# Centroid similarities of a clustered attention: centroids as stationary operand in four column groups instead of queries and keys

## What is computed

```
q_assign = argmax(q_n . c_n)      # per token, over 16 centroids; k_assign the same for keys
mask     = q_assign[i] == k_assign[j]
scores   = where(mask, scale * q k^T, -1e9)
attn     = softmax(scores);   out = attn v
```

## Time and profile before

| what | value |
|---|---|
| median of three runs | 680.38 us (678.81 to 681.3) |
| the profiled execution, its own time | 680.13 us |
| its span, first to last instruction | 678.3 us |
| mean granted TensorE clock | 0.995 of full speed |
| TensorE matmuls busy (PE) | 661.5 us, 98% |
| TensorE weight loads busy (PEld) | 635.9 us, 94% |
| VectorE busy (DVE) | 382.3 us, 56% |
| ScalarE busy (ACT) | 321.7 us, 47% |
| GpSimd busy (POOL) | 191.7 us, 28% |

### The profile page before, as it was taken

One profiled execution on the slowest core, in us unless ns is written; L12 is line 12 of the kernel. 1 busy time (PEld: TensorE's weight loads), 2 busy tenths in 40 slices (PEclk: granted clock), 3 DMA queues, 4 the chain that ended last, 5 costly groups with the idle time before them and its releaser, 6 DMA issues.

```text
span 678.3 us, 11306 instructions
## 1 busy us (share of the span) xinstructions
PE 661.5 (98%) x4050; PEld 635.9 (94%) x4050; DVE 382.3 (56%) x650; ACT 321.7 (47%) x619; POOL 191.7 (28%) x140
## 2 busy tenths in 40 slices
PE   7899899999999998999999999999999999999998
PEld 6889799999999997889999999999999999999997
DVE  6889798989899895443212212312378336661142
ACT  4787778787787884344202102202478125520010
POOL 5568254554525854106200000200243000060000
PEclk8999999999999999999999999999999999999999
DMA  6584745537473611102100000100421000000022
GB/s 217 104 196 127 182 101 119 144 76 173 79 185 79 145 47 47 47 0 94 63 1 0 1 1 0 46 0 1 140 86 55 16 1 1 1 1 1 0 94 94
DMA packets 16976, 46.92 MB, mean 69 GB/s; under 512 B 3024, under 2 KB 5072, under 8 KB 16944
## 3 DMA queue, kind: packets, MB, share of 16 engines
q1 hardware_dynamic: 16944, 46.48, 25.9%
HBM read 24.15 MB, written 3.15 MB: 40 GB/s over the span
## 4 chain that ended last, share of the span: by engine, by line
PE 95%; DVE 2%; ACT 1%; DMA 1%; issue 1%; SPq 0%
PE ps L459 20%; PE ps L457 20%; PE ps L458 20%; PE ps L497 9%; PE ps L505 5%; PE ps L489 5%; PE ps L506 5%; PE ps L490 5%; PE ps L471 3%; PE ps L512 2%; DMA kb<-oh_rows 1%; PE ps L707 1%; PE ps L480 1%; PE ps L640 1%; ACT x_t L780 0%
## 5 line engine op out<-in xcount | busy, mean ns | idle before, releaser
L780 ACT ACTIVATE pt_hi<-ps 128x384 fp32r<-128x384 f32 x192 | 85.0, 489 | 42.9 <-PE ps L497 42.0
L1100 DVE TENSOR_TENSOR pt_lo<-ps,pt_hi 128x384 fp32r<-128x384 f32 x192 | 97.3, 548 | 9.6 <-ACT pt_hi L780 8.3
L1073 DVE TENSOR_REDUCE neg_max<-ps 128x1 f32<-128x768 f32 x96 | 91.1, 950 | 20.0 <-PE ps L490 19.4
L811 ACT ACTIVATE prob<-ps,neg_max 128x768 f32<-128x768 f32 x96 | 86.8, 904 | 6.3 <-DVE neg_max L1073 6.3
L894 ACT ACTIVATE g_s<-ps 128x384 fp32r<-128x384 f32 x48 | 23.6, 492 | 138.9 <-PE ps L459 138.9
L459 PE MATMUL ps<-u_s,ch_s 128*128 128x384 f32 (+1 forms) x256 | 85.5, 334 | 0.0
L457 PE MATMUL ps<-u_s,ch_s 128*128 128x384 f32 (+1 forms) x256 | 85.5, 334 | 0.0
L458 PE MATMUL ps<-u_s,ch_s 128*128 128x384 f32 (+1 forms) x256 | 85.5, 334 | 0.0
L497 PE MATMUL ps<-ident,prob 128*128 128x128 f32 x576 | 82.4, 277 | 0.5 <-DVE pt_lo L1100 0.4
L497 PEld LDWEIGHTS ps<-ident,prob 128*128 128x128 f32 x576 | 66.5, 142 | 10.0 <-issue 2.3
L489 PE MATMUL ps<-ka,qa 128*128 128x384 f32 x192 | 70.9, 369 | 5.1 <-DMA kb<-oh_rows 3.0
(11 more groups left out here) (147 smaller groups left out, 1374.0 us busy)
## 6 DMA issues: line engine op xcount, KB each, us to landing
stage<-ch_dram SPq DMA_DIRECT2D x9, 768.0 KB, 4.4
qa<-pair_s SPq DMA_DIRECT2D x30, 192.0 KB, 3.0
ka<-pair_s SPq DMA_DIRECT2D x30, 192.0 KB, 4.0
raw<-q_dram SPq DMA_DIRECT2D x8, 384.0 KB, 4.4
raw<-k_dram SPq DMA_DIRECT2D x8, 384.0 KB, 4.6
raw_v<-v_dram SPq DMA_DIRECT2D x8, 384.0 KB, 4.3
out_dram<-act_u SPq DMA_DIRECT2D x16, 192.0 KB, 1.9
qb<-pair_s SPq DMA_DIRECT2D x15, 192.0 KB, 3.4
```

What stands on the lines that cost most here:

```text
L780: return act.activation(o, i, ACT.Copy)
L811: act.activation(prob[:, slot, :].rearrange("p (c k) -> p c k", c=2), ps[:, 2 * slot:2 * slot + 2, 0:HS], ACT.Exp, bias=neg_max[:, s:s + 1 ...
L1073: dve.tensor_reduce(neg_max[:, s:s + 1], ps[:, 2 * slot2:2 * slot2 + 2, 0:HS], AX.XY, ALU.max, negate=True).then_inc(s_max, 1)
L1100: dve.tensor_tensor(pt_lo[at], ps[:, 4 + u, 0:HS].rearrange("p (k q) -> p k q", k=HT), pt_hi[at], ALU.subtract).then_inc(s_pt_lo, 1)
```

## The change

The similarities of a pair are computed with the centroids as the stationary operand (32 columns) and the queries or keys as moving operand (384 columns). Four such matmuls make up a pair: two sides, two halves of the tokens. Each writes its own 32 partitions of bank 7, and so uses its own group of 32 columns of the array. The result is centroid by token; ScalarE copies it to `sim_rows`, and three transposes bring it back to token by centroid in bank 7. The matmuls go to step 0 and the transposes to step 1, both behind what TensorE does there. [...] Argmax number 0 moves to step 1, numbers 1 and 2 stay in step 3. The one-hot rows are ordered by side first and then by head, so the setup has four small memsets where it had eight. Pair 0's own similarities at the start keep their form, with other addresses.

```diff
+                cen_p = sb(a1, "cen_p", [P, 2 * C], F32)
+                sim_rows = sb(a1, "sim_rows", [P, HS], F32)
...
             def oh_in(p, j):
...
-                    r = j * D + side * 2 * C
+                    r = side * D + j * 2 * C
...
+            def centroids_of(p, first=False):
+                if not first:
+                    pool.wait_ge(s_cen_t, 4)
+                    pool.wait_ge(s_sim_pe, p - 1)
+                pool.tensor_tensor(cen_p[:], cen_t[:].rearrange("p b c -> p (b c)")[:, bass.ds(p * 2 * C, 2 * C)],
+                                   one[:].broadcast_to([P, 2 * C]), ALU.mult).then_inc(s_cen_p, 1)
...
                 if scaled:
                     scale_q(p + 2)
+                    centroids_of(p + 2)
...
             scale_q(1)
+            pool.wait_ge(s_cen_t, 2)
+            centroids_of(1, first=True)
             split_v(0, 0, first=True)
...
-            def sims(p, side, src=raw, bank=7, first=False):
-
-                if side == 0 and not first:
-                    pe.wait_ge(s_oh_rows, p)
-                    pe.wait_ge(s_cen_t, 4)
-                    pe.wait_ge(s_qk_c, p)
-                groups = ps[:, bank, 0:24 * C].rearrange("p (t j s c) -> p t j s c", t=NT, j=2, s=2)
-                centroids = cen_t[:].rearrange("p b c -> p (b c)")[:, bass.ds(p * 2 * C, 2 * C)]
-                for t in range(NT):
-                    mm = pe.matmul(groups[:, t, :, side, :], src[:, side, t * P:(t + 1) * P],
-                                   centroids.rearrange("p (j c) -> p j c", j=2), start=True, stop=True)
-                if side == 1 or first:
-                    mm.then_inc(s_sims, 1)
+            def sims(p):
+
+                pe.wait_ge(s_oh_rows, p)
+                pe.wait_ge(s_cen_p, p)
+                pe.wait_ge(s_qk_c, p)
+                for side in range(2):
+                    for half in range(2):
+                        r = (2 * half + side) * 2 * C
+                        mm = pe.matmul(ps[r:r + 2 * C, 7, 0:HS], cen_p[:], raw[:, side, half * HS:(half + 1) * HS],
+                                       start=True, stop=True)
+                mm.then_inc(s_sim_pe, 1)
+
+            def sims_transpose(p):
+
+                pe.wait_ge(s_sim_rows, p)
+                for t in range(HT):
+                    mm = pe.transpose(ps[:, 7, t * P:(t + 1) * P], sim_rows[:, t * P:(t + 1) * P], ident[:])
+                mm.then_inc(s_sims, 1)
...
-                    if s == 3 and not last:
-                        sims(p + 1, 0)
+                    if s == 0 and not last:
+                        sims(p + 1)
...
-                    if s == 3 and not last:
-                        sims(p + 1, 1)
+                    if s == 1 and not last:
+                        sims_transpose(p + 1)
...
+                    if s == 0 and not last:
+                        act.wait_ge(s_sim_pe, p + 1)
+                        copy(sim_rows[:], ps[:, 7, 0:HS]).then_inc(s_sim_rows, 1)
                     if s == 7 and not last:
...
                     if not last:
-                        for step in {3: (0, 1, 2), 4: (3,), 6: (4,)}.get(s, ()):
+                        for step in {1: (0,), 3: (1, 2), 4: (3,), 6: (4,)}.get(s, ()):
                             argmax(p + 1, step)
```

More of the change, by code:

```diff
@@ L80, in clustered_mixer @@
                 pt_lo = sb(a1, "pt_lo", [P, 2, NT, HS], F32R)
-                onehot = sb(a1, "onehot", [P, NT, 2, 2, 2 * C], BF16)
+                onehot = sb(a1, "onehot", [P, HT, 2, 2, 2, 2 * C], BF16)
                 oh_rows = sb(a1, "oh_rows", [P, S], F32R)
@@ L137, in clustered_mixer @@
         s_cen_t = sem("s_cen_t")
+        s_cen_p = sem("s_cen_p")
+        s_sim_pe = sem("s_sim_pe")
+        s_sim_rows = sem("s_sim_rows")
         s_sims = sem("s_sims")
@@ L459, in product, with sims_first @@
                 return pe.matmul(o, a_hi, b_hi, start=False, stop=stop)
-            def sims(p, side, src=raw, bank=7, first=False):
-                if side == 0 and not first:
-                    pe.wait_ge(s_oh_rows, p)
-                    pe.wait_ge(s_cen_t, 4)
-                    pe.wait_ge(s_qk_c, p)
-                groups = ps[:, bank, 0:24 * C].rearrange("p (t j s c) -> p t j s c", t=NT, j=2, s=2)
-                centroids = cen_t[:].rearrange("p b c -> p (b c)")[:, bass.ds(p * 2 * C, 2 * C)]
-                for t in range(NT):
-                    mm = pe.matmul(groups[:, t, :, side, :], src[:, side, t * P:(t + 1) * P],
-                                   centroids.rearrange("p (j c) -> p j c", j=2), start=True, stop=True)
-                if side == 1 or first:
-                    mm.then_inc(s_sims, 1)
+            def sims_first(side, bank):
+                groups = ps[:, bank, 0:24 * C].rearrange("p (t h s j c) -> p t h s j c", t=HT, s=2, h=2, j=2)
+                for t in range(NT):
+                    mm = pe.matmul(groups[:, t % HT, t // HT, side, :, :], raw0[:, side, t * P:(t + 1) * P],
+                                   cen_t[:, 0, 0:2 * C].rearrange("p (j c) -> p j c", j=2), start=True, stop=True)
+                mm.then_inc(s_sims, 1)
[13 more added lines that the diff above has]
+                    mm = pe.transpose(ps[:, 7, t * P:(t + 1) * P], sim_rows[:, t * P:(t + 1) * P], ident[:])
+                mm.then_inc(s_sims, 1)
             def oh_transpose(bank=7):
@@ L480, in oh_transpose @@
                     mm = pe.transpose(rows[:, t * P:(t + 1) * P],
-                                      onehot[:, t, :, :, :].rearrange("p j s c -> p (j s c)"), identb[:])
+                                      onehot[:, t % HT, t // HT, :, :, :].rearrange("p s j c -> p (s j c)"), identb[:])
                 mm.then_inc(s_oh_t, 1)
@@ L594, in _ @@
             pe.wait_ge(s_q0_scaled, 1)
-            sims(0, 0, src=raw0, first=True)
+            sims_first(0, bank=7)
             pe.wait_ge(s_raw_k0, 16)
-            sims(0, 1, src=raw0, bank=4, first=True)
+            sims_first(1, bank=4)
             for side in range(2):
@@ L799, in mask_rows_first @@
                 act.wait_ge(s_oh_t, 2)
-                act.activation(kb[D:D + C, 0, :], ps[2 * C:3 * C, 5, 0:HS].bitcast(BF16), ACT.Copy,
+                act.activation(kb[D:D + C, 0, :], ps[D:D + C, 5, 0:HS].bitcast(BF16), ACT.Copy,
                                scale=BIG, bias=-BIG).then_inc(s_koh, 1)
@@ L842, in pair @@
                         rows_out(p + 1)
-            act.wait_ge(s_oh_zero, 9)
+            act.wait_ge(s_oh_zero, 5)
             query_rows_first()
@@ L985, in _ @@
             dve.memset(onehot[:], 0.0).then_inc(s_oh_zero, 1)
[L986 to L989, removed]
+            for side in range(2):
+                rows = slice(side * D, (side + 1) * D)
+                dve.memset(oh_scale[rows, :], BIG if side else 1.0).then_inc(s_oh_zero, 1)
+                dve.memset(oh_bias[rows, :], -BIG if side else 0.0).then_inc(s_oh_zero, 1)
             for c in range(C):
@@ L1025, in _ @@
             normalised(1, 1)
-            hot = onehot[:].rearrange("p t j s c -> p (t j) s c")
+            hot = onehot[:].rearrange("p t h s j c -> p (t h) s j c")
             def argmax_first(side):
-                r = slice(12 * side, 12 * side + 12)
-                sim = ps[:, 4 if side else 7, 0:24 * C].rearrange("p (n s c) -> p n s c", s=2, c=C)[:, :, side, :]
-                shape = [P, 12, C]
+                at1, at2 = (m[:].rearrange("p (s t n) -> p s t n", s=2, t=NT)[:, side] for m in (am1, am2))
+                sim = ps[:, 4 if side else 7, 0:24 * C].rearrange("p (t s n c) -> p t s n c", t=NT, s=2, c=C)[:, :, side]
+                shape = [P, NT, 2, C]
                 dve.wait_ge(s_sims, side + 1)
-                dve.tensor_reduce(am1[:, r], sim, AX.X, ALU.max).then_inc(s_am0, 1)
+                dve.tensor_reduce(at1, sim, AX.X, ALU.max).then_inc(s_am0, 1)
                 dve.wait_ge(s_am0, 4 * side + 1)
-                dve.tensor_tensor(sim, sim, am1[:, r].unsqueeze(2).broadcast_to(shape),
+                dve.tensor_tensor(sim, sim, at1.unsqueeze(3).broadcast_to(shape),
                                   ALU.is_ge).then_inc(s_am0, 1)
                 dve.wait_ge(s_am0, 4 * side + 2)
-                dve.tensor_tensor(sim, sim, order[:].unsqueeze(1).broadcast_to(shape),
+                dve.tensor_tensor(sim, sim, order[:].unsqueeze(1).unsqueeze(1).broadcast_to(shape),
                                   ALU.mult).then_inc(s_am0, 1)
                 dve.wait_ge(s_am0, 4 * side + 3)
-                dve.tensor_reduce(am2[:, r], sim, AX.X, ALU.max).then_inc(s_am0, 1)
+                dve.tensor_reduce(at2, sim, AX.X, ALU.max).then_inc(s_am0, 1)
                 dve.wait_ge(s_am0, 4 * side + 4)
@@ L1045, in argmax_first @@
                     dve.wait_ge(s_oh_t, 1)
-                dve.tensor_tensor(hot[:, :, side, 0:C], sim, am2[:, r].unsqueeze(2).broadcast_to(shape),
```

(3 more changed lines are left out.)

## The result

| what | before | after |
|---|---|---|
| median of six runs each | 680.84 us (678.81 to 682.61) | **676.22 us** (675.06 to 677.14) |
| the profiled execution, its own time | 680.13 us | 675.06 us |
| its span | 678.3 us | 673.3 us |
| mean granted TensorE clock | 0.995 | 0.997 |

What follows compares the result with a forecast made beforehand. TensorE, at 98% of the span, and VectorE were both taken as full in steps 3 to 7. Pair 0's 0.63, pair 1's 0.25 and 2.60 for pairs 2 to 6 gave +3.5 on 680.13: 683.6 us, range 676.6 to 690.0.

Steps and rivals of the forecast that it cites:

- the price of the new matmuls: Step 0 on TensorE: four new similarity matmuls of two records each, put at 1.84 us a pair with changing over.
- a staircase of five records: Step 0: only the next matmul's first record overlaps, 5 x 0.35 = 1.75 us; the chosen case, chance 0.45.
- X: Time the new similarities hold TensorE in step 0 of a pair: 1.84 us, with 0.79 and 2.89 as alternatives.
- The price of a record: Each new matmul leaves two records on TensorE, each between 0.18 and 0.35 us; the upper value was taken.
- The changing over: Step 0: the first matmul after transposes holds the next back 0.26 us, not 0.18, so 0.09 was added.
- The pair's sum: One steady pair, step 0 to step 8: from 20.46 us to 19.14 + X, a change of +0.52 us.
- the prediction's main reading: Steps 3 to 7: both engines are full and VectorE is behind; removing the old similarities, 2.52 us, uncovers it.
- Waits for low parts: TensorE in steps 5 and 6: waits rise from nearly none to some 0.5 us in each pair.
- The gaps on VectorE: From row maximum to one-hot rows: waits of 0.69, 0.14 and 0.16 us go, leaving steps without a gap.
- all at once: Step 0: all four matmuls overlap, X = 0.79, -0.53 a pair, 677.3 us; its family's chance 0.30.
- Pair 1: Its end waits 3.03 us for the one-hot rows' DMA; its own delay is swallowed, GpSimd's copy adds 0.25.
- At nothing: Parts costed at no time: ScalarE's copy of 0.50 us, the one-hot rows' new order and the shorter setup memsets.

Runs made afterwards that it cites:

- two groups in a row: The changed kernel with the two similarity matmuls of each side in the same column group, one side's two before the other's; 680.51 us.
- number 1 early: The changed kernel with argmax number 1 moved from step 3 to step 1, behind number 0; 673.98 us, ratio 0.9906.
- number 2 doubled: The changed kernel with argmax number 2 of step 3 executed twice; 679.74 us, ratio 0.999.
- one-group kernel: The changed kernel with all four similarity matmuls of a pair writing the same 32 partitions, so using the same 32 columns; 686.5 us.
- in turns: The changed kernel with two column groups, each used by one side's two matmuls, the sides alternating in program order; 679.0 us.

## Why the prediction was wrong

**The step that failed** is the price of the new matmuls. The prediction took "a staircase of five records", on the ground that "only the next matmul's first record can run beside it", X = 1.84 us. Measured: 0.87, all four side by side. The kernel with two groups in a row shows that a matmul doesn't even wait for the start of one ahead of it in another group. The evidence for a staircase was that matmuls of the trace start in program order, but every one of those uses all the columns of the array: it could not speak of groups. This one term is worth 6 x 0.97 = 5.8 us; with 0.87 in its place the same sum gives 677.8.

**The price of a record** was right: 0.32 us for 0.35. The changing over was taken as 0.09; the way in costs 0.09 and the way out 0.76 - 2 x 0.32 = 0.12. The Trainium skill (TensorEngine Tiling (Array Packing), Key Properties) says that a change of tiling mode drains the engine. Whether it does can't be read from the rows; the way in and the way out together cost 0.2 us in them, not the 0.32 that the prediction set beside it.

**The pair's sum** held. With X = 0.87 the formula gives X - 1.32 = -0.45 a pair; -0.67 was measured. The difference is in VectorE's stretch, 11.74 for 11.97: behind argmax number 3 the row maximum before had waited 0.64 - 0.47 = 0.17 us more, a wait too short for a bracket in the timeline, and it too went. That VectorE, not TensorE, pays for what is in steps 3 to 6 was the prediction's main reading, and the kernels with number 1 early and number 2 doubled confirm it by -0.53 and +0.56.

**Waits for low parts** up by "some 0.5 us in each pair": the rows of the weight loads have 1.5 more, of which 0.6 lie behind the similarities and cost TensorE nothing. In the one-group kernel, where X is 1.9 us longer, they are 1.1 in all, so the waits of steps 2 to 6 don't hang on X. What came back as waiting in all is about 0.65 us, for the 0.9 predicted; that difference is VectorE's shorter stretch again. The gaps on VectorE went, as said.

**The rival "all at once"** had the mechanism, a chance of 0.30, and 677.3 us. Against it the change came 1.1 us better in the median and 2.2 in the profiled executions: 5 x 0.14 for the pairs (-0.67 for -0.53), pair 1 and the noise of the start. Given the mechanism the size was good; the choice between the cases was not.

**Pair 1** was wrong in detail, and right in the main point. "Over 3 us late, no stall" was read in pair 2, and in pair 1 `cen_p` is late and TensorE waits 0.85 us. Nor was the clash of the addition with GpSimd seen. Both were swallowed, as the prediction said of all that pair 1 does: its end came 0.64 us earlier instead of 0.25 later, as the wait of 3.03 us fell to 0.23.

**At nothing** were costed the order of the one-hot rows and the memsets (shown: 0.999), ScalarE's copy (0.50 us in the rows and nobody waits for it) and GpSimd's copy, which took 0.24 us for the 0.25 assumed.

## What to carry to other kernels

When a matmul has few stationary columns, put independent ones into different column groups: here the array charged only for the fullest group, even where the program had them one group after another. When two engines are nearly level, the cheap lever is which of them holds an instruction in the stretch where it is behind: moving one VectorE instruction of 0.59 us two steps earlier gave 0.53 us a pair, nearly the 0.67 of the whole change. And read every exceptional pass of a loop by itself: waits in the first pairs were unlike the steady ones, and a DMA at their end took back what was gained there.

## What was unexpected of the hardware

Column groups don't wait for each other: with two matmuls in one group ahead of two in another, the four took 1.42 us, as in turns (1.41). Three matmuls more in free groups cost 0.02 us.

A VectorE addition of six numbers per partition, from SBUF to SBUF, was held for 3.36 us, to the end of a GpSimd instruction that had begun 0.15 us before it. In the other kernels that have it the longest took between 0.47 and 3.42 us, for a usual 0.16, and each time it ended within 0.04 us of the end of a GpSimd instruction. A reciprocal of the same size under the same kind of GpSimd instruction was not (0.18 us). The Trainium skill (SBUF — State Buffer, Who interferes with whom) says that VectorE's additions with a constant can take a pair of ports shared with GpSimd, and that who is first keeps it for the whole instruction; these rows agree. That it is the ports, and not something else that the two engines share, no run here shows.
